# GpSimd's head-preparation work laid out anew between its scaling pairs in a clustered-attention kernel

## The reference

```
q_assign = argmax(q_n @ c_n.T)          # 2 x 8 heads, 768 rows of 64, 16 clusters
k_assign = argmax(k_n @ c_n.T)
mask     = q_assign[:, None] == k_assign[None, :]
scores   = where(mask, q @ k.T / 8, -1e9)
attn     = exp(scores - max(scores)); attn = attn / (sum(attn) + 1e-9)
x        = attn @ v                     # laid out as 1536 tokens x 512
h = x @ w_in;  g = P(h) / Q(h);   x = g @ w_out      # first feed-forward, 512 -> 2048 -> 512
h = x @ w2_in; g = h - tanh(h); out = g @ w2_out     # second feed-forward
```

## Time and profile before

| | us |
|---|---|
| median of three runs | 822.67 (822.06 to 823.25) |
| time of the profiled execution | 823.63 |
| its span, first to last instruction | 821.8 |
| busy in the span: PE, DVE, ACT, POOL | 791.9, 526.7, 501.5, 353.0 |
| attention part, tile 0 to tile 95 | from about 25 to 291 |

### The profile page before, as it was taken

How to read it: one execution, slowest core, us unless ns; L and a number is a source line. 1 busy time by engine, 2 the same in 40 slices (tenths; PEclk the granted TensorE clock), 3 DMA queues, 4 the chain that set the end, 5 groups by cost and what they waited for, 6 DMA issues and landing times.

```text
span 821.8 us, 11654 instructions
## 1 busy us (share of the span) xinstructions
PE 791.9 (96%) x4066; PEld 680.3 (83%) x4066; DVE 526.7 (64%) x910; ACT 501.5 (61%) x954; POOL 353.0 (43%) x377
## 2 busy tenths in 40 slices
PE   5899999999999899999999999999999999999998
PEld 5789998989898787888788888888888888888886
DVE  4599889898988879999977787995311211111111
ACT  3578788888888877878776777777422222222222
POOL 5467787877877723213222222226622222222222
PEclk7699999999999999999999999999999999999999
DMA  4723323332330205200000011115100100001001
GB/s 129 188 72 76 85 73 83 85 77 72 83 74 19 68 11 154 77 0 1 1 0 1 1 51 52 52 52 170 35 1 1 51 1 1 0 9 44 1 0 52
DMA packets 39082, 41.17 MB, mean 50 GB/s; under 512 B 4720, under 2 KB 30320, under 8 KB 39024
## 3 DMA queue, kind: packets, MB, share of 16 engines
q1 hardware_dynamic: 39024, 40.42, 17.5%
HBM read 26.25 MB, written 3.15 MB: 36 GB/s over the span
## 4 chain that ended last, share of the span: by engine, by line
PE 55%; POOL 20%; DVE 13%; issue 6%; ACT 3%; SPq 2%; DMA 1%; POOLq 0%; DVEq 0%; ACTq 0%
PE y_ps L1060 27%; PE h_ps L1039 25%; POOL probs L407 9%; DVE f_bc L841 2%; DVE f_t L860 2%; DVE w_lo L815 2%; DVE f_bc L858 2%; POOL nq L416 2%; DVE f_a L854 2%; POOL v L433 1%; POOL nk L424 1%; POOL hot L441 1%; POOL x_lo L452 1%; DVE f_t L846 1%; POOL hot L442 1%
## 5 line engine op out<-in xcount | busy, mean ns | idle before, releaser
L498 POOL TENSOR_TENSOR g_lo<-f_t,g_hi 128x512 fp32r<-128x512 f32 x96 | 125.1, 1303 | 377.7 <-ACT g_hi L594 377.7
L897 DVE TENSOR_TENSOR f_t<-h_ps,f_a 128x512 f32<-128x512 f32 x48 | 33.2, 691 | 203.4 <-ACT f_a L673 203.4
L1039 PE MATMUL h_ps<-x_hi,w_hi 128*128 128x512 f32 x384 | 149.5, 389 | 1.3 <-DVE w_lo L815 1.3
L1039 PE MATMUL h_ps<-x_lo,w_hi 128*128 128x512 f32 x384 | 149.5, 389 | 0.0
L1039 PE MATMUL h_ps<-x_hi,w_lo 128*128 128x512 f32 x384 | 149.4, 389 | 0.0
L594 ACT ACTIVATE g_hi<-f_t 128x512 fp32r<-128x512 f32 x96 | 60.8, 633 | 138.8 <-PE y_ps L1060 123.4
L407 POOL TENSOR_SCALAR probs<-probs,rinv 128x768 f32<-128x768 f32 x96 | 86.3, 911 | 69.2 <-DVE rinv L782 65.9
L557 ACT ACTIVATE pt_hi<-pt_ps 128x384 fp32r<-128x384 f32 x192 | 85.3, 492 | 48.3 <-PE pt_ps L979 47.1
L788 DVE TENSOR_TENSOR pt_lo<-pt_ps,pt_hi 128x384 fp32r<-128x384 f32 x192 | 98.5, 547 | 13.8 <-ACT pt_hi L557 13.1
L775 DVE TENSOR_REDUCE nmax<-s_ps 128x1 f32<-128x768 f32 x96 | 91.0, 948 | 7.4 <-PE s_ps L966 6.5
L979 PE MATMUL pt_ps<-ident,probs 128*128 128x128 f32 x576 | 85.1, 283 | 6.7 <-POOL probs L407 5.6
(11 more groups left out here) (122 smaller groups left out, 1571.7 us busy)
## 6 DMA issues: line engine op xcount, KB each, us to landing
w_raw<-in_moe_w_in_dram SPq DMA_DIRECT2D x32, 256.0 KB, 2.9
w_raw<-in_moe_w_out_dram SPq DMA_DIRECT2D x32, 256.0 KB, 3.7
ka<-qk_b SPq DMA_DIRECT2D x32, 192.0 KB, 3.0
raw_q<-in_q_dram SPq DMA_DIRECT2D x16, 192.0 KB, 2.6
raw_k<-in_k_dram SPq DMA_DIRECT2D x16, 192.0 KB, 2.9
raw_v<-in_v_dram SPq DMA_DIRECT2D x16, 192.0 KB, 3.1
qk_b<-qa SPq DMA_DIRECT2D x16, 192.0 KB, 2.7
out_dram<-f_bc SPq DMA_DIRECT2D x12, 256.0 KB, 2.1
```

The source lines that it names most:

```text
L498: pool.tensor_tensor(g_lo[n % 2][:, :], f_t[n % 2][:, :], g_hi[n % 2][:, :].bitcast(F32), ALU.subtract).then_inc(g_lo_done, 1)
L897: dve.tensor_tensor(f_t[n % 2][:, :], h_ps[n % 4][:, :], f_a[n % 2][:, :], ALU.subtract).then_inc(g_done, 1)
L1039: last = pe.matmul(h_ps[n % 4][:, :], w[f][:, ws], x[:, cols], start=(kt == 0 and i == 0), stop=(kt == KT - 1 and i == 2))
```

## The change

Three jobs move, and what depends on them.

```diff
@@ GpSimd's loop @@
-                if r == 1 and 3 <= (k + 17) // T < HEADS:
-                    split_k((k + 17) // T)
-                if r == 2 and 2 <= (k + 10) // T < HEADS:
-                    rank_hot((k + 10) // T)
+                if k == 1:
+                    split_k(FIRST + 1)
+                if r == 1 and 2 <= (k + 11) // T < HEADS:
+                    rank_hot((k + 11) // T)
                 if r == 3 and 1 <= (k + 3) // T < HEADS:
                     split_v((k + 3) // T)
+                if r == 3 and FIRST + 2 <= (k + 21) // T < HEADS:
+                    split_k((k + 21) // T)
@@ SyncE ahead of its loop, behind load_v(1) @@
+            sp.wait_ge(k_split, 2)
+            load_k(4)
@@ SyncE's loop @@
-                if (k + 15) % T == 0 and 4 <= (k + 15) // T + 1 < HEADS:
-                    g = (k + 15) // T + 1
+                if (k + 27) % T == 0 and 5 <= (k + 27) // T < HEADS:
+                    g = (k + 27) // T
@@ the weight chunks @@
-        ACT_CHUNK_AT = {78: 0, 80: 1, 84: 2, 88: 3, 94: 4}
-        POOL_CHUNK_AT = {79: 0, 83: 1, 85: 2, 91: 3}
+        ACT_CHUNK_AT = {74: 0, 80: 1, 84: 2, 88: 3, 94: 4}
+        POOL_CHUNK_AT = {77: 0, 83: 1, 85: 2, 91: 3}
```

## The result

The changed kernel takes 831.23 us (median of 4 runs, 828.78 to 831.49) against 822.6: a ratio of 1.0098, 95% interval 1.0078 to 1.0118. Timed again without an edit it gave 830.79 and 1.0096 (1.0078 to 1.0115). Its profiled execution took 828.78 us, a span of 827.0, 5.2 more than that of before.

What follows compares the result with a forecast made beforehand. No engine full, two near it, so the order of waits decides. 5.55 + 0.4 + 0.2 + 0.6 - 0.1 = 6.65, say 6.7 us, takes the median from 822.67 to 829.4; range 824.2 to 832.6.

Steps and rivals of the forecast that it cites:

- The step-4 wait goes: TensorE's step-4 transposes stop waiting for GpSimd's scalings, 0.78 us in head 6 and 0.59 in head 7.
- VectorE is held: In step 3, L755 is blocked by GpSimd's rest of the values: 0.55 us in head 6, 0.70 in head 7.
- VectorE isn't held: Rival: head 0's 0.99 us has another cause or VectorE comes first each time; 822.3, no change; chance 0.08.
- the waits go and nothing is behind them: Rival: twelve waits at step 4 vanish and VectorE's list closes up, 8.2 us saved, 815.1; chance 0.09.
- held in even heads only: Rival: VectorE is blocked only in even heads, each step costs about half, 826.0 or a little under; chance 0.07.
- In head 0: L755 is held there already, but L757 is free and will meet the keys: +0.2 us.
- a case that I had named for odd heads: In step 3 of odd heads, VectorE comes first and L757 is held instead of L755, about 0.25 us.
- From there to TensorE: VectorE's delay reaches TensorE, +0.56 us odd to even heads, +0.55 even to odd; five pairs give 5.55, head 1 +0.4.
- GpSimd's new wait: The wait of `split_k` for TensorE's second key unit, behind step 4's transposes, costs nothing.
- SyncE, +0.6: At the start, one key load ahead of the weights and `spread_hot` delays them: +0.6 us (0 to 0.8).
- The end, -0.1: Moved weight chunk delays head 13's step 0 by 0.9 to 1.3 us, step 1 regains 1.4: net -0.1.
- The clock: Rival: stalls of about 0.95 us ahead of step 5 drop TensorE to 1.2 GHz; 838 or 855 us; chance 0.03.

Runs made afterwards that it cites:

- the gate: Changed kernel with GpSimd's rest of the values made to wait until VectorE's `hot_nat` of step 3 is done: 823.52 us, 1.0004 against the kernel before.
- the kernel with less work: Kernel before with the key splits of heads 3 to 15 left out, one column of `nk` set instead: 827.41 us, 1.0054 against the kernel before.
- the second version with and without its gate: Changed kernel with GpSimd's wait, old chunk places, keys split in even heads only, `x_low`'s second half behind the queries, `load_k(4)` later: 821.52 us; without the wait 828.84 us.
- the loads alone: Kernel before with only SyncE's part of the change, key loads moved earlier: 822.94 us, 0.9997 against the kernel before.
- the chunk put back: Changed kernel with the first weight chunk where it was, ScalarE in tile 78 and GpSimd in tile 79: 830.13 us, 1.0091 against the kernel before.
- the kernel with the memset: Changed kernel with GpSimd's rest of the values replaced by writing zeros to the same tensor: 824.33 us, 1.0017 against the kernel before.

## Why the prediction was right

It said 829.4 (824.2 to 832.6) and slower at 0.83; the time is 831.2. The profiled execution was to take 830.3; three of them took 828.8, 831.9 and 828.5. The sum of 6.65 was 1.2 to 1.5 us more than the traces show (5.2 to 5.4) and 0.8 to 1.9 us less than the medians do (7.5 to 8.6), so that the median came within 2 us is in part luck; the mechanism isn't. Three slips carry little: the 0.05 us for a signal stands in no row, the bounds named add up to 825.6 and 832.0, not 826.0 and 832.5, and "no engine is full" passes over PE, TensorE's multiplication, at 48.68 us of 50 in the earlier trace rows. By its own steps:

- **The step-4 wait goes.** It does: 9.7 us for scalings are 1.3.
- **VectorE is held.** L759 takes 0.77 us in head 6, so it costs 0.51 more (predicted 0.53), and 0.95 in head 7, 0.70 more (predicted 0.77). This step decided the result: the gate, the kernel with less work and the second version with and without its gate all turn on it, and each moves the time by 4.5 to 7.3 us. "VectorE isn't held", "the waits go and nothing is behind them" and "held in even heads only" are ruled out by these rows.
- **In head 0** VectorE came first, a case that I had named for odd heads. The changed kernel's rows:

```profile
44.48 0.41 DVE L759 TENSOR_TENSOR hot_nat<-hot,top 128x96 f32<-128x96 f32 x1
44.92 1.02 DVE L761 TENSOR_SCALAR hot_nat<-hot_nat 128x96 f32<-128x96 f32 x1
```

  L435 runs there from 44.86 to 45.87, and now L761 is the one that is held, until 45.94: five times its 0.21 us. I had priced that case at 0.25. Here L761 loses 0.81 and L759 gains 0.58 (0.41, not 0.99): together +0.23, where I had +0.2 for another reason.
- **From there to TensorE.** From `rinv` of step 2 of head 6 to that of head 7 it is 159.46 - 142.54 = 16.92 us, against 156.34 - 139.86 = 16.48: +0.44, predicted +0.55. From head 7 to head 8 it is 16.70, against 16.13: +0.57, predicted +0.56. Together 1.01 for these two heads and 1.04 on average, predicted 1.11. Five of them gave 5.18 in the first pair of traces and 5.37 in the second, predicted 5.55. The path into odd heads was told a little wrong: I expected the queries' wait to grow to near 1 us. It is 0.44 (from 0.38), because TensorE itself comes later by the 1.02 us it now waits at step 5. The sum is the same by either way.
- **GpSimd's new wait** for TensorE's key unit: there is no such wait in the trace, and behind the keys GpSimd still idles 1.39 us.
- **SyncE, +0.6.** Not shown. In a kernel of its own the time moved by -1.2 to +0.7 us, the issue wasn't later, and TensorE waited last for `qa`. In the three traces of the changed kernel the six DMAs end 0.3 to 0.9 us later than in the two of before; whether that passes in full to TensorE stays open. Up to tile 14 (SyncE, head 0 and head 1, together 1.2) the first pair of traces gives +0.60, the second -0.73. That stretch varies more than these terms, and they aren't settled one by one.
- **The end, -0.1.** Right in sum, and partly by luck. From tile 74 to 94 the first pair of traces gives -0.62, the second +0.75. The part up to tile 80 came as predicted (+1.14 and +1.17, predicted 0.9 to 1.3). The gain of 1.4 behind it came out as 1.76 in the first pair and 0.42 in the second. I had read it off a trace in which TensorE's granted clock fell in just that place. The transposes of step 5 of head 13 in the first trace of before, then in its second:

```profile
259.85 1.26 PEld L979 LDWEIGHTS pt_ps<-ident,probs 128*128 128x128 f32 x6
```

```profile
259.74 0.71 PEld L979 LDWEIGHTS pt_ps<-ident,probs 128*128 128x128 f32 x6 [0.16 <-issue]
```

  The fall isn't rare, though: of the seven traces with the chunk in tiles 78 and 79 (two of the kernel before, and those of the loads alone, of less work, of the chunk put back and of the second version with and without its gate) five have one between 252 and 268 us, of the six with it moved none. How much of the gain most runs get is open.
- **The clock.** That rival was wrong where I put it: over the heads the clock stays at 1.00 in spite of waits of 1.02 us. But the median of the changed kernel lies 7.5 to 8.6 us above that of before, and the traces of 828.8 and 828.5 us explain only 5.2 to 5.4. The trace of 831.9 us has the rest. Its windows (granted clock behind the counts), then TensorE behind the wait, and the same window of the trace of 828.8:

```profile
40.00:44.00 4.00, 3.28 (x14) 3.21 (x15) 1.65 (x4) 1.34 (x4) 1.81 (x3) 0.61 0.39 98
292.00:296.00 4.00, 2.69 (x8) 2.42 (x9) 2.00 (x5) 0.95 (x3) 2.18 (x3) 0.68 0.71 217
```

```profile
293.28 0.19 PEld L1000 LDWEIGHTS pv_ps<-pt_hi,v 128*128 128x128 f32 x1 [1.56 <-issue]
293.39 0.26 PEld L1000 LDWEIGHTS pv_ps<-pt_lo,v 128*128 128x128 f32 x1
293.64 0.33 PEld L1000 LDWEIGHTS pv_ps<-pt_hi,v 128*128 128x128 f32 x1
```

```profile
292.00:296.00 4.00, 4.00 (x23) 3.44 (x23) 0.54 (x2) 0.17 (x1) 1.03 (x2) 1.00 0.37 125
```

  Behind a wait of 1.56 us a load of 0.19 us takes 0.33, the lower level of 1.2 GHz. Its stretch from tile 94 to the end takes 537.3 us instead of 535.8. It comes to tile 14 1.3 us later than the first trace (72.46 against 71.19), with a fall at 40 to 44 us; the first has one of its own there, at 20 to 36 us, and the third (828.5 us) has none and is at tile 14 at 70.84. These 1.3 and 1.5, with 0.25 between tiles 14 and 74, are the 3.1 us between the spans. The unchanged kernel has such falls too, as at 259.85 above, and the same wait of 1.56 us without a fall behind it. Whether the changed one has them more often, and so the 2 to 3 us by which the median is further off than the traces, stays open: runs without a profile show only a mean clock, and that doesn't follow their time.

The Trainium skill ("SBUF — State Buffer", section "Who interferes with whom") says that of a VectorE instruction with two SBUF inputs and a GpSimd instruction that reads SBUF the second to start is blocked for the whole of the first. The traces agree for L759 (0.77 and 0.95 us, ending 0.1 us behind GpSimd) and for the gate (0.25 with GpSimd idle), and `pt_lo`, with one input in PSUM, keeps its 1.01 us for two halves beside GpSimd's split of the keys. For GpSimd's copy in the kernel with the memset they agree only in part: it shares 0.23 us with `hot_nat`, which started first, and is 0.09 us longer.

## What to carry to other kernels

Taking an engine's lateness away also moves all that stands behind it on that engine, to a new place against the others. Before such a move, lay the timelines of GpSimd and VectorE on each other and look which instruction of VectorE with its inputs in SBUF will now fall into one of GpSimd's, small ones too (128x2 was held 2.35 us); an idle wait of 1.2 us on GpSimd that keeps them apart was worth 7 us here. And trace the kernel before twice ahead of pricing a step of 1 us: one of my terms was read off a place where the clock had fallen in that trace and not in the next.

## What the runs showed of the hardware

- VectorE's form with one tensor input (L761, 128x96) is held as well: 0.40 us beside GpSimd's copy and 1.02 us beside its L435, against 0.21 alone. I had expected that for the copy, from the earlier trace rows, and not that it could be held for a whole microsecond.
- A very small instruction of VectorE can be held as well: `rsum_e` on 128x2 took 2.35 us instead of 0.16 beside GpSimd's split of a 128x1024 chunk, in all three kernels that have the keys out of the gap and the chunk in its old place (the changed one with the chunk back, the second version with and without its gate). It isn't always so: in the kernel before it started at 156.00, 0.13 us into GpSimd's L441, and took 0.23.
- This kernel lost 4.5 us (1.0054) by having less to do on an engine that isn't full.
- TensorE's granted clock stays at 1.00 over eleven heads with a wait of 1.0 us in each. Behind the same wait of 1.56 us it fell in one of three traces of the changed kernel and stayed at 1.00 in the others, and the fall cost 1.5 us (537.3 against 535.8).
